# Three layers in one kernel: expert rows read in sorted order, gated at PSUM, and stored by index

## The reference, cut to what matters

```python
def _moe_ref(x, w_gate, w_output_gate, w1, w2):      # x [1536, 512], w1 [8, 512, 1024], w2 [8, 1024, 512]
    logits = x @ w_gate
    e_idx = np.argmax(logits, axis=1)
    ...                                               # gate_w: softmax probability of the chosen expert
    eom = 1.0 / (1.0 + np.exp(-(x @ w_output_gate)))
    for e in range(E):
        mask = e_idx == e
        h = np.maximum(x[mask] @ w1[e], 0.0)
        ye = h @ w2[e]
        out[mask] = gate_w[mask, None] * eom[mask, e, None] * ye
    return out

def _moe2_ref(x, w_in, w_out):                        # w_in [512, 2048], w_out [2048, 512]
    h = x @ w_in
    g = np.where(h > 0.0, h, np.exp(np.minimum(h, 0.0)) - 1.0)
    return g @ w_out
```

## Time and profile before

| | us |
|---|---|
| median of 3 runs (lowest, highest) | 861.65 (859.6, 862.1) |
| the profiled execution's own time | 866.3 |
| its span in the trace | 864.5 |
| TensorE busy | 800.7, 93% of the span |
| VectorE, ScalarE, GpSimd busy | 464.6, 376.5, 309.1 |
| mean granted TensorE clock | 0.968 |

### The profile page before, as it was taken

How to read it: one execution, slowest core, us unless ns; L and a number is a source line. 1 busy time by engine, 2 the same in 40 slices (tenths; PEclk the granted TensorE clock), 3 DMA queues, 4 the chain that set the end, 5 groups by cost and what they waited for, 6 DMA issues and landing times.

```text
span 864.5 us, 12964 instructions
## 1 busy us (share of the span) xinstructions
PE 800.7 (93%) x4445; PEld 676.7 (78%) x4445; DVE 464.6 (54%) x805; ACT 376.5 (44%) x711; POOL 309.1 (36%) x244
## 2 busy tenths in 40 slices
PE   4999999999999749899999999839989999999998
PEld 3787878778776537588888888729969988988986
DVE  4777777787787445344444444415923632731740
ACT  2777777777776412222333330004712711720630
POOL 4142333435443149678877775012440010000000
PEclk9999999999999959899999999968999999999999
DMA  5032223111100056755666540340020010000000
GB/s 171 30 101 74 72 76 100 38 47 47 37 10 19 20 181 211 230 180 176 215 219 207 178 163 26 120 148 1 1 85 25 2 49 25 1 13 25 1 13 25
DMA packets 41565, 72.67 MB, mean 84 GB/s; under 512 B 17888, under 2 KB 24160, under 8 KB 41504
## 3 DMA queue, kind: packets, MB, share of 16 engines
q10 hardware_dynamic: 10240, 33.56, 11.4%
q1 hardware_dynamic: 28784, 30.16, 10.8%
q0 software_dynamic: 2480, 8.13, 3.3%
HBM read 60.56 MB, written 11.27 MB: 83 GB/s over the span
## 4 chain that ended last, share of the span: by engine, by line
PE 80%; DVE 6%; DMA 4%; another core or an unknown queue 3%; ACT 3%; POOL 2%; issue 1%; ACTq 1%; SPq 1%; DVEq 0%
PE pair_t L1137 14%; PE pair_t L1074 10%; PE pair_s L1061 10%; PE bank_b L970 8%; PE pair_s L1125 7%; PE pair_u L951 7%; PE pair_u L1125 6%; PE pair_s L940 4%; PE pair_t L940 4%; PE bank_a L917 3%; PE bank_a L890 2%; PE bank_b L981 2%; PE pair_u L1043 1%; POOL w_part L397 1%
## 5 line engine op out<-in xcount | busy, mean ns | idle before, releaser
L397 POOL TENSOR_TENSOR w_part<-w_raw,w_part 128x1024 fp32r<-128x1024 f32 x80 | 189.7, 2410 | 79.3 <-ACT w_part L544 79.3
L544 ACT ACTIVATE w_part<-w_raw 128x1024 fp32r<-128x1024 f32 x72 | 71.4, 1049 | 152.2 <-issue 129.4
L1061 PE MATMUL pair_s<-w_part,xs_t 128*128 x456 | 114.7, 406 | 6.6 <-issue 4.1
L1137 PE MATMUL pair_t<-w_part,g_hi 128*128 128x512 f32 x384 | 119.1, 391 | 1.4 <-POOL w_part L397 1.4
L1074 PE MATMUL pair_t<-w_part,hid_t 128*128 x456 | 110.5, 398 | 2.6 <-DVE hid_t L808 2.6
L1061 PEld LDWEIGHTS pair_s<-w_part,xs_t 128*128 128x128 f32 x456 | 87.6, 196 | 26.9 <-issue 9.3
L1074 PEld LDWEIGHTS pair_t<-w_part,hid_t 128*128 128x128 f32 x456 | 85.5, 191 | 20.5 <-issue 2.8
L1137 PEld LDWEIGHTS pair_t<-w_part,g_hi 128*128 128x128 f32 x384 | 71.6, 188 | 16.2 <-issue 1.8
L951 PE MATMUL pair_u<-ident_r,exps 128*128 128x128 f32 x576 | 79.2, 273 | 3.0 <-DVE exps_t L682 2.6
L1137 PE MATMUL pair_t<-w_part,g_lo 128*128 128x512 f32 x192 | 74.9, 390 | 0.0
L951 PEld LDWEIGHTS pair_u<-ident_r,exps 128*128 128x128 f32 x576 | 68.4, 140 | 7.9 <-DVE exps_t L682 3.3
(11 more groups left out here) (139 smaller groups left out, 1219.0 us busy)
## 6 DMA issues: line engine op xcount, KB each, us to landing
w_raw<-in_moe_w ACTq DMA_DIRECT2D x48, 512.0 KB, 4.8
w_raw<-in_moe_w SPq DMA_DIRECT2D x16, 512.0 KB, 5.2
ys_sorted<-ys SPq DMA_DIRECT2D x19, 256.0 KB, 5.4
w_raw<-in_moe_w_in ACTq DMA_DIRECT2D x8, 512.0 KB, 4.6
w_raw<-in_moe_w_out ACTq DMA_DIRECT2D x8, 512.0 KB, 5.0
raw<-in_q SPq DMA_DIRECT2D x16, 192.0 KB, 2.4
raw<-in_k SPq DMA_DIRECT2D x16, 192.0 KB, 2.7
v_nat<-in_v SPq DMA_DIRECT2D x16, 192.0 KB, 2.4
```

The source lines that it names most:

```text
L397: pool.tensor_tensor(chunk_of(w_part, n, 1, c), w_raw[n % 2][c][:, :], chunk_of(w_part, n, 0, c).bitcast(F32), ALU.subtract).then_inc(s_wl ...
L544: act.activation(chunk_of(w_part, n, 0, c), w_raw[n % 2][c][:, :], ACT.Copy).then_inc(s_whi, 1)
L1061: mm = pe.matmul(pair_s[:, h, :], xs_t[:, xp, c * P:(c + 1) * P], w_part[:, bass.ds(par, 1), wp, a:a + 512], start=c == 0 and n == 0, stop ...
L1137: mm = pe.matmul(pair_t[:, t % 2, :], gp[:, f, j * P:(j + 1) * P], w_out_p[:, wp, f, :], start=f == 0 and m == 0, stop=f == FT - 1 and m == 2)
```

## The change

The dense layers take rows in sorted order. Tile t holds the sorted rows 128t to 128t+127 without the padding: seven new small instructions on VectorE compute `row_at`, where each of them stands in `ys_sorted`. Since the padding before a row is less than 8 slots, tile t needs slots 0 to t+7 alone, and each gather waits for those. The first three gathers stand before the low parts of set 8, the next three before those of set 9, and all later ones a block ahead. The gate is brought to the sorted order as three bf16 parts (three multiplications on GpSimd, 12 small matmuls and a reduction in slot 0) and applied when `copy_y` reads PSUM. `copy_y` also writes each place's row number as a 513th column, in an instruction of its own; after the gather it is copied to `token`, and GpSimd stores each finished output tile by those indices, in place of SyncE's plain store. `scale_y` is gone. TensorE turns the first two tiles of block 0 before `layer2(17)` and the third after `turn_h(18)`, and VectorE writes both parts of them there. The wait for the last `copy_y` moves from ahead of block 0 to ahead of its second layer. Four chunks of `w_out` are converted as soon as they land, before ScalarE waits for the end of the last slot's layer 2; the other four after column groups 6, 8, 10 and 12. Rows in `x_rows` are laid out in output order.

```diff
--- before.py
+++ after.py
@@ -60,6 +60,8 @@
+YW = DM + 1
+GP = 3
...
     put("rev", np.tile(E - np.arange(E), TILES))
-    put("tiles128", np.tile(P * np.arange(TILES), E))
+    put("tiles128", np.tile(np.concatenate([[-1], P * np.arange(1, TILES)]), E))
     put("upto", (np.arange(E)[None, :] <= np.arange(E)[:, None]).astype(np.float32).ravel())
...
     put("starts", np.tile(P * np.arange(SLOTS + 1), TILES))
-    token = TILES * np.arange(P)[:, None] + np.repeat(np.arange(TILES), SLOTS)[None, :]
+    tile = np.repeat(np.arange(TILES), SLOTS)[None, :]
+    token = S * (tile // J) + J * np.arange(P)[:, None] + tile % J
     put("eights", token // 8 * 8)
...
     put("iota", np.arange(P))
+    put("row", P * np.arange(TILES)[None, :] + np.arange(P)[:, None])
     put("alt", np.tile(1.0 - 2.0 * (np.arange(E - 1) % 2), SLOTS))
...
@@ -119,14 +123,15 @@
         sem = lambda n: ctx.enter_context(nc.semaphore(n))
-        x_dram = nc.dram_tensor("x_rows", [P * TILES, DM], F32).ap()
-        ys_dram = nc.dram_tensor("ys_sorted", [SLOTS * P, DM], F32).ap()
+        x_dram = nc.dram_tensor("x_rows", [TOK, DM], F32).ap()
+        ys_dram = nc.dram_tensor("ys_sorted", [SLOTS * P, YW], F32).ap()
...
         ident_r = keep("ident_r", [P, P], F32R)
-        gate = keep("gate", [P, TILES])
-        pos = keep("pos", [P, TILES], U32)
+        gate_slot = keep("gate_slot", [P, SLOTS])
+        row_at = keep("row_at", [P, TILES], U32)
+        token = keep("token", [P, TILES], U32)
         src = keep("src", [P, SLOTS], U32)
...
@@ -383,10 +402,6 @@
-            for t in range(TILES):
-                sp.wait_ge(s_o, t + 1)
-                sp.dma_start(out.rearrange("(b p j) d -> b p j d", b=B, j=J)[t // J, :, t % J, :],
-                             o_sb[:, :]).then_inc(s_od, 16)
             sp.wait_ge(s_od, 16 * TILES)
@@ -466,28 +481,52 @@
                 gather_x(s)
+            pool.wait_ge(s_parts, 1)
+            for i in range(GP):
+                pool.tensor_tensor(place_g[:, :, i, :], in_slot[:, :, :],
+                                   gate_bf[:, i, :].unsqueeze(2).broadcast_to([P, TILES, SLOTS]),
+                                   ALU.mult).then_inc(s_gplace, 1)
             for c in range(NCH):
...
                 gather_x(s)
-            for n in range(2, E + 1):
+            for n in range(2, E):
                 for c in range(NCH):
...
             def gather(t):
+                last = min(t + E - 1, SLOTS - 1)
+                for i in range(2):
+                    pool.wait_ge(s_yst[i], 16 * ((last - i) // 2 + 1))
                 if t >= BT:
-                    pool.wait_ge(s_ysp, t - BT + 1)
-                pool.indirect_dma_start(y_raw[:, t % BT, :], None, ys_dram,
-                                        bass.IndirectOffsetOnAxis(pos[:, t:t + 1], 0)).then_inc(s_yg[t % BT], 16)
-            for i in range(2):
-                pool.wait_ge(s_yst[i], 16 * ((SLOTS + 1 - i) // 2))
+                    pool.wait_ge(s_yt, t - BT + 1)
+                    pool.wait_ge(s_tok, t - BT + 1)
+                pool.indirect_dma_start(y_raw[:, t % BT, :], None, ys_dram[0:(last + 1) * P, :],
+                                        bass.IndirectOffsetOnAxis(row_at[:, t:t + 1], 0)).then_inc(s_yg[t % BT], 16)
+            def scatter(t):
+                pool.wait_ge(s_tok, t + 1)
+                pool.wait_ge(s_o, t + 1)
+                pool.indirect_dma_start(out, bass.IndirectOffsetOnAxis(token[:, t:t + 1], 0),
+                                        o_sb[:, :], None).then_inc(s_od, 16)
+            pool.wait_ge(s_row, 1)
             for t in range(BT):
...
             for c in range(NCH):
+                w_lo(E, c)
+            for t in range(BT, 2 * BT):
+                gather(t)
+            for c in range(NCH):
                 w_lo(E + 1, c)
-            for t in range(BT, TILES):
-                gather(t)
+            for blk in range(BLOCKS):
+                for j in range(BT):
+                    scatter(blk * BT + j)
+                    if blk + 2 < BLOCKS:
+                        for i in TURN_AFTER[j]:
+                            gather((blk + 2) * BT + i)
...
@@ -578,6 +617,9 @@
                             wait_release(act, n, c, ends)
+                        if n == E + 1 and c == NC1:
+                            for i in range(NC1):
+                                w_hi(n, i)
                         act.dma_start(chunk_dst(n, c), chunk_source(n, c)).then_inc(s_wld[c], 16)
...
@@ -585,11 +627,10 @@
             for blk in range(BLOCKS):
-                for j in range(BT):
+                for j in range(BT if blk >= 1 else 0):
                     t = blk * BT + j
                     act.wait_ge(s_yt, t + 1)
-                    if blk >= 1:
-                        act.wait_ge(s_f1, FT * blk)
+                    act.wait_ge(s_f1, FT * blk)
                     act.activation(y_t[:, 0, :, j * P:(j + 1) * P], ring[t % 2].rearrange("p (c n) -> p c n", c=CD),
...
@@ -605,8 +646,8 @@
                         act.activation(g_hi[:, f - 1, :], elu[:, n % 3, :], ACT.Copy).then_inc(s_gh, 1)
-                        if blk == 0 and f % 2 == 0:
-                            w_hi(E + 1, f // 2 - 1)
+                        if blk == 0 and f >= NC1 + 2 and f % 2 == 0 and f // 2 + 1 < NCH:
+                            w_hi(E + 1, f // 2 + 1)
...
@@ -756,7 +797,7 @@
                 dve.tensor_scalar(at_row[:, t, :], iota_bf[:, :], r_m[:, t:t + 1], None, ALU.is_equal).then_inc(s_at, 1)
-            dve.tensor_copy(pos[:, :], r_f[:, :]).then_inc(s_pos, 1)
+            dve.tensor_copy(counts[:, :], rank[:, TILES, :]).then_inc(s_cnt, 1)
...
@@ -778,7 +819,24 @@
             then(dve.reciprocal(r_z[:, :], r_z[:, :]))
-            dve.tensor_tensor(gate[:, :], r_p[:, :], r_z[:, :], ALU.mult).then_inc(s_gate, 1)
+            then(dve.tensor_tensor(gate[:, :], r_p[:, :], r_z[:, :], ALU.mult))
+            for i in range(GP - 1):
+                then(dve.tensor_copy(gate_bf[:, i, :], gate[:, :]))
+                then(dve.tensor_tensor(gate[:, :], gate[:, :], gate_bf[:, i, :], ALU.subtract))
+            dve.tensor_copy(gate_bf[:, GP - 1, :], gate[:, :]).then_inc(s_parts, 1)
+            dve.wait_ge(s_cnt, 1)
+            then(dve.tensor_tensor(up, counts[:, :].unsqueeze(1).broadcast_to([P, E, E]),
+                                   cc("upto").rearrange("p (e f) -> p e f", e=E), ALU.mult))
+            then(dve.tensor_reduce(c_end[:, :], up, AX.X, ALU.add))
+            then(dve.scalar_tensor_tensor(pad[:, :], n_tile[:, :], float(P), counts[:, :], ALU.mult, ALU.subtract))
+            then(dve.tensor_tensor(past[:, :, :], cc("row").unsqueeze(2).broadcast_to([P, TILES, E]),
+                                   c_end[:, :].unsqueeze(1).broadcast_to([P, TILES, E]), ALU.is_ge))
+            then(dve.tensor_tensor(past[:, :, :], past[:, :, :], pad[:, :].unsqueeze(1).broadcast_to([P, TILES, E]),
+                                   ALU.mult))
+            then(dve.tensor_reduce(shift[:, :], past[:, :, :], AX.X, ALU.add))
+            dve.tensor_tensor(row_at[:, :], cc("row"), shift[:, :], ALU.add).then_inc(s_row, 1)
...
@@ -812,27 +870,47 @@
                 dve.wait_ge(s_l2, s + 2)
-                dve.tensor_copy(ys[:, s % 2, :], pair_t[:, s % 2, :]).then_inc(s_y, 1)
-            dve.wait_ge(s_gate, 1)
+                dve.tensor_copy(ys[:, s % 2, DM:YW].bitcast(U32), src[:, s:s + 1])
+                dve.tensor_scalar(ys[:, s % 2, 0:DM], pair_t[:, s % 2, :], gate_slot[:, s:s + 1], None,
+                                  ALU.mult).then_inc(s_y, 1)
+            def gates():
+                dve.wait_ge(s_gtok, 1)
+                dve.tensor_reduce(gate_slot[:, :], pair_t[:, 1, 0:GP * SLOTS].rearrange("p (i s) -> p s i", i=GP),
+                                  AX.X, ALU.add).then_inc(s_gslot, 1)
+            def take_yt(t):
+                to = slice(t * P, (t + 1) * P)
+                turned = ring[t % 2].rearrange("p (c n) -> p c n", c=CD)
+                dve.wait_ge(s_yt, t + 1)
+                dve.tensor_copy(y_t[:, 0, :, to], turned).then_inc(s_yte, 1)
+                dve.wait_ge(s_yte, t + 1)
+                dve.tensor_tensor(y_t[:, 1, :, to], turned, y_t[:, 0, :, to].bitcast(F32),
+                                  ALU.subtract).then_inc(s_yte_lo, 1)
+                keep_token(t)
+            def keep_token(t):
+                dve.wait_ge(s_yg[t % BT], 16 * (t // BT + 1))
+                dve.tensor_copy(token[:, t:t + 1], y_raw[:, t % BT, DM:YW].bitcast(U32)).then_inc(s_tok, 1)
             copy_xt(0)
...
                     copy_xt(s + 1)
+                if s == 0:
+                    gates()
+                    dve.wait_ge(s_gslot, 1)
+                if s == SLOTS - 1:
+                    take_yt(0)
+                    take_yt(1)
                 if s < SLOTS:
...
                     copy_y(s - 1)
-            def scale_y(t):
-                j = t % BT
-                if t >= BT:
```

(85 more changed lines are left out.)

## The result

| | us |
|---|---|
| kernel before, median of 4 runs | 861.88 (859.6 to 862.12) |
| changed kernel, median of 4 runs | 847.54 (845.45 to 849.12) |
| ratio | 0.9838 (95%: 0.9809 to 0.9867) |
| profiled execution of the changed kernel: time, span | 848.45, 846.6 |

I had forecast 839 with a range of 834 to 845.5. The direction was right; 14.3 us came of the 22.6 forecast.

What follows compares the result with a forecast made beforehand. The prediction took TensorE, busy 93% of the span, as the bound and sought its waits. Its terms, -17.00 - 7.51 + 0.3 + 1.6 = -22.6 us, taken from 861.65, gave 839.05, predicted as 839, range 834 to 845.5.

Steps and rivals of the forecast that it cites:

- the tail: End of the span: the last tile's indexed store lands later than SyncE's plain one, +1.6 us, bounds 0.3 and 4.6.
- VectorE's term: Block 0: VectorE's steps held up beside GpSimd's low parts, +0.3 us, bounds 0 and 4.
- The hole, -17.00: Ahead of block 0: TensorE's wait goes, block 0 following layer2(18) at 568.26 instead of 585.26, 17.00 us saved.
- Block 0, -7.51: Block 0 was to lose its 7.51 us over block 1: slow clock, wait for a low part, late gather.
- rival 1: Block 0 is paced by VectorE: 4 us stay, 843 us; chance 0.10.
- Rivals 4 and 5: Dense layers: a 13.2 us scatter uses up the gain (0.03); a tile awaits the last slot's store, 17 us back (0.03).
- When `w_out` is converted: Four chunks converted from about 556 us, GpSimd's low parts from about 564 to 574; the other four between 582 and 598.
- The added work before, 0: Before block 0: new small instructions, gathers, one-column copies in copy_y and 513th column fit into idle time, cost 0.
- The scatter, +1.6: Tile stores by index cost only at the end: landing 3.6 us after issue against 2.0, +1.6 us.
- Rival 2: A stall like TensorE's 4.07 us pause in slot 3 appears elsewhere, 4 to 8 us: 843 to 847; chance 0.14.
- Rival 3: The clock doesn't drop in layer2(18) after a shorter wait: 1.6 us go, 837.4 is left; chance 0.10.

Runs made afterwards that it cites:

- after_split: The changed kernel with GpSimd making the first four low parts of set 2 before the last four gathers of expert rows: 842.04 us, ratio 0.9768.
- after_plain_store: The changed kernel with SyncE's plain store of each tile in place of GpSimd's indexed one, output left in sorted order: 844.52 us, ratio 0.9795.
- after_rel0: The changed kernel with ys moved and 1,984 unused bytes, so the other operands lie a multiple of 2,048 bytes from w_part: 839.84 us, again 839.44.
- after_rel0_split: The changed kernel with the edits of after_rel0 and after_split together: 834.30 us, ratio 0.9687.
- before_pad96: The kernel before with 96 unused bytes per partition behind slot_tab, no instruction changed: 861.02 us, ratio 1.0002.
- after_best: The changed kernel with the edits of after_rel0_split and w_out's first four chunks converted before ScalarE's wait for the last layer 2: 840.80 us, again 836.08.
- before_gap32: The kernel before with 32 unused bytes per partition between the weight area and the tensors above it, one run: 872.94 us (before 867.13).
- before_gap256: The kernel before with 256 unused bytes per partition between the weight area and the tensors above it, one run: 866.81 us (before 867.13).
- before_gap1024: The kernel before with 1,024 unused bytes per partition behind the weight area, in the slots alone, one run: 864.47 us (before 867.13).
- after_gap32: The changed kernel with 32 unused bytes per partition between the weight area and the tensors above it: 848.52 us, ratio 0.9869.
- after_pad32: The changed kernel with 32 unused bytes per partition behind slot_tab, no instruction changed: 848.17 us, ratio 0.9862.
- after_same: The changed kernel itself, run again: 846.08 us, ratio 0.9826.

## Why the prediction was wrong

**The step that failed** is the one that carried TensorE's durations over: "block 1 lasts 727.81 - 660.29 = 67.52 us, with the same matmuls and turns", and the sum, which has no term for the matmuls of the slots and of the dense layers at all. They were the same instructions, and they got longer, because the change laid tensors with 513 columns between the weights and the other operands. The size follows from the links: 38 layers in the slots at 5.60 in place of 5.48 us are 4.6 us, 12 tiles at 11.19 in place of 10.93 are 3.1, and eight pairs of groups in block 0 at 4.24 in place of 4.16 are 0.6, together 8.3 us. The last 0.6 is not shown to be the layout's: after_split and after_plain_store have the changed kernel's layout and 4.16 us there. after_rel0 got 7.7 back and landed at 839.84 and 839.44, against the 839.05 of my sum (840.1 with the tail and VectorE's term put right, see below). The layout was in the diff (`YW = DM + 1`, and the new order of `sb` lines); I read it as lifetimes only, and gave no chance to a rival in which equal instructions change their time.

The other terms:
- *The hole, -17.00.* Right, by mechanism and size: the turns stand at 550 us ahead of `layer2(17)`, the third in the wait of TensorE, and block 0 follows without a gap. Only the absolute time of its start is luck, as said above.
- *Block 0, -7.51.* Right: without the layout's part it is 67.5 us in after_rel0_split too (its first tile starts 33.3 us after block 0's start, and a tile takes 10.93). TensorE never waited for VectorE, so my 0.3 us were 0 and rival 1 did not come. Rivals 4 and 5 did not come either: no tile waited for a scatter, and nothing stands between `layer2(18)` and block 0.
- *When `w_out` is converted.* Wrong in a point that cost nothing, and the section on the change has it wrong as well: the four conversions stand behind ScalarE's wait for the last layer 2, not ahead of it. They ran at 567.97, and GpSimd's low parts at 569.11, not 564, beside the ELU of block 0.
- *The added work before, 0.* Right. The one-column copies in `copy_y`, from the trace's summary of that line (min, median and max ns of 19):

```profile
L873 DVE COPY ys<-src x19: 144/146/155, 341.2 to 568.0; 128x1 uint32<-128x1 uint32 x19
```

  No copy was held up, though 11 of the 19 began while GpSimd made a low part, so the case that I had taken from the Trainium skill's rule (GPSIMD Engine Reference, Key points) cost nothing. The copy has one input; a step with two, `g_lo` at 594.44, again took 2.79 us beside a low part.
- *The scatter, +1.6.* That only the last one costs was right, the size was half: 3.0 us. It landed in 2.7 us, 0.7 more than a plain store and 0.9 less than a gather, but it starts about 0.7 us later behind the copy, and the span ends about 1.7 us later behind its landing. The sum had a term for neither.
- *Rival 2.* The pause is not in every execution of the program, but it hit the profiled one of before. In the same place before_pad96, with the instructions of before, has ScalarE's issue at 350.39 in place of 360.30:

```profile
350.39 2.24 ACTq L582 DMA_DIRECT2D w_raw<-in_moe_w  x4
```

  TensorE's pauses are gone there too. I had held that nothing is won when TensorE's pause goes; ScalarE's went with it, and slot 4 begins 5.6 us earlier than at 372.87:

```profile
367.25 7.35 PE L1062 MATMUL pair_s<-w_part,xs_t 128*128 x24 [3.71 <-POOL w_part L398]
```

  It runs at the low clock there, so 4.0 us are left by slot 5 (381.44 against 385.47), of the 4.65 us by which the profiled execution lay above its median. Taking the change from the median was right for that reason, which I did not know. What causes the pause was not tried. It shows in 5 of the 18 traces, with ScalarE's issue between 355.01 and 360.38: the one of the kernel before, and all four from the chip on which the kernel before took 867.13 us (after_best, before_gap32, before_gap256, before_gap1024). So it seems to go with a chip or its state and not with the program.
- *Rival 3.* The clock fell in `layer2(18)` of the changed kernel's trace, as I had taken it. But it did not in those of after_split, after_plain_store, after_gap32, before_gap256 and before_gap32 (5.70 to 5.88 us behind waits of 2.14 to 2.63). So the shorter wait did not decide it; it is worth about 1.5 us whichever way it falls, before the change and after it, and is part of the spread of the timed runs.

In sum: 839.05 + 8.3 (longer matmuls) + 1.4 (tail) - 0.3 (VectorE) = 848.5 against 847.54 measured. The 1.0 us left is less than one fall of the clock.

## What to carry to other kernels

When a change moves or resizes tensors, TensorE's durations of before are not safe to carry over: compare the same group of matmuls in both traces before anything else, since 2.2 to 2.4% on each was more than half of what this change brought. Keep the two operands of such matmuls a multiple of 256 bytes apart in SBUF, and put tensors of odd width where they shift nothing. A short wait of TensorE can cost more than its length (2.44 us cost 4.0 here) when the granted clock falls behind it, which it does not always do. A burst of indirect DMAs on GpSimd ahead of work that TensorE needs is worth splitting.

## What the runs showed of the hardware

- Back-to-back 512-column float32r matmuls, each with its own 128x128 weights, follow each other in 227.9 ns on average (most in 226 or 227) when the two operands' distance in SBUF is a multiple of 256 bytes (0, 256 and 1,024 tried). When it is off by 32, 64, 96 or 128 bytes the mean is 233.2, 233.4, 233.9 and 232.4. The first step of each 24 is left out of these means. Whether the operands start 0 or 32 bytes past a multiple of 64 made no difference to them. That it is a conflict between reading the moving operand and the next weights is my guess; only the layout was shown.
- 384-column matmuls took, at the full clock, 173.3 to 173.5 ns at a distance of 0 or 64, and 175.5 at 128. At 32 both 173.3 and 176.7 occur: 176.7 in every block of after_pad32 and in blocks 1 to 3 of before_gap32, but in the changed kernel and after_same only in block 0, and in after_split and after_plain_store, with the same layout, in no block. So here the distance alone does not decide, and what does stays open.
- An indirect store of 128 rows of 2 KB landed 2.7 us after its issue, a plain one 2.0. As the last work of the kernel it put the end of the span 5.5 us behind the last copy, the plain one 2.5.
- Behind a wait of TensorE of 2.1 to 2.7 us the granted clock fell to 0.77 or 0.78 in some traces and stayed at 1.00 in others, also with the same instructions and the same wait: 24 matmuls took 7.2 to 7.5 us or 5.7 to 5.9.
